# Four units of a gated convolution multiply behind the gathered rows, in quarters instead of halves

## The reference

```
h = np.maximum(x @ w_in, 0.0)                 # x: (2, 768, 384), w_in: (384, 1024)
conv_out[t] = sum over k of conv_w[k] * h[t + k - 1]     # 3 taps, zero-padded
gate = 1.0 / (1.0 + np.exp(-conv_out))
out  = (h * gate) @ w_out                     # w_out: (1024, 384)
```

## Time and profile before

| | us |
|---|---|
| median of 3 runs | 523.26 (516.58 to 534.95) |
| the profiled execution | 522.37 |
| its span, first to last instruction | 520.9 |
| TensorE busy in the span | 484.9 (93%) |
| DVE, ACT, POOL busy | 375.4, 288.2, 82.4 |

### The profile page before, as it was taken

How to read it: one execution, slowest core, us unless ns; L and a number is a source line. 1 busy time by engine, 2 the same in 40 slices (tenths; PEclk the granted TensorE clock), 3 DMA queues, 4 the chain that set the end, 5 groups by cost and what they waited for, 6 DMA issues and landing times.

```text
span 520.9 us, 15282 instructions
## 1 busy us (share of the span) xinstructions
PE 484.9 (93%) x6083; PEld 424.1 (81%) x6083; DVE 375.4 (72%) x606; ACT 288.2 (55%) x469; POOL 82.4 (16%) x121
## 2 busy tenths in 40 slices
PE   8979999999999888899999999999986699999997
PEld 4548888687677657799989989999876689999997
DVE  6887787676024344999999999999875467789661
ACT  4513443241123241999899899898853254444543
POOL 6622232020201121010010110100004400000000
PEclk9979999799579688899999999999997799999999
DMA  7672301022420105485476476430163300000202
GB/s 142 119 135 41 65 6 35 4 53 82 143 81 19 49 30 183 152 287 190 149 271 209 151 254 213 164 107 30 62 226 89 109 0 1 2 0 1 91 2 91
DMA packets 59275, 52.58 MB, mean 101 GB/s; under 512 B 41395, under 2 KB 52275, under 8 KB 59094
## 3 DMA queue, kind: packets, MB, share of 16 engines
q1 hardware_dynamic: 53142, 39.21, 26.0%
q0 software_dynamic: 3968, 12.19, 6.8%
q10 hardware_dynamic: 2112, 0.39, 0.4%
HBM read 77.74 MB, written 10.22 MB: 169 GB/s over the span
## 4 chain that ended last, share of the span: by engine, by line
PE 81%; DVE 6%; SPq 4%; issue 4%; DMA 2%; ACT 2%; another core or an unknown queue 1%; DVEq 0%; ACTq 0%
PE ps L1916 5%; PE ps L1918 5%; PE ps L1917 5%; PE ps L1130 5%; PE ps L1934 5%; PE ps L1933 5%; PE ps L1935 5%; PE ps L2199 3%; PE ps L2201 3%; PE ps L2213 3%; PE ps L2214 3%; PE ps L2215 3%; PE ps L2200 3%; PE ps L1291 3%; PE ps L1925 3%
## 5 line engine op out<-in xcount | busy, mean ns | idle before, releaser
L1837 DVE TENSOR_TENSOR w2l<-raw,w2h 128x768 fp32r<-128x768 f32 x76 | 67.7, 953 | 6.8 <-ACT w2h L1770 6.8
L1837 DVE TENSOR_TENSOR w1l<-raw,w1h 128x1024 fp32r<-128x1024 f32 x57 | 66.4, 1220 | 6.3 <-ACT w1h L1770 4.3
L1770 ACT CAST w1h<-raw 128x1024 fp32r<-128x1024 f32 x57 | 56.4, 1063 | 4.7 <-DMA raw<-in_moe_w_dram 4.7
L1770 ACT CAST w2h<-raw 128x768 fp32r<-128x768 f32 x76 | 58.1, 848 | 0.2 <-DMA raw<-in_moe_w_dram 0.2
L1933 PE MATMUL ps<-w2h,hh 128*128 128x384 f32 x152 | 52.4, 345 | 1.6 <-DVE hl L1842 1.6
L1935 PE MATMUL ps<-w2h,hl 128*128 128x384 f32 x152 | 50.9, 335 | 0.0
L1934 PE MATMUL ps<-w2l,hh 128*128 128x384 f32 x152 | 50.8, 334 | 0.0
L1130 PE MATMUL ps<-idle_b 128*128 128x512 bf16 (+3 forms) x160 | 47.1, 402 | 1.9 <-DVE idle_b L765 1.8
L1916 PE MATMUL ps<-w1h,xh 128*128 128x512 f32 x114 | 47.0, 412 | 0.6 <-DVE xl L1829 0.6
L1918 PE MATMUL ps<-w1h,xl 128*128 128x512 f32 x114 | 45.2, 397 | 0.0
L1917 PE MATMUL ps<-w1l,xh 128*128 128x512 f32 x114 | 44.8, 393 | 0.0
(11 more groups left out here) (232 smaller groups left out, 1046.5 us busy)
## 6 DMA issues: line engine op xcount, KB each, us to landing
raw<-in_moe_w_dram SPq DMA_DIRECT2D x54, 512.0 KB
raw<-in_moe_w_dram SPq DMA_DIRECT2D x72, 384.0 KB
x_all<-x_sorted POOLq DMA_DIRECT2D x19, 192.0 KB, 2.9
y_sorted<-x_all POOLq DMA_DIRECT2D x19, 192.0 KB, 2.6
raw<-in_q_dram SPq DMA_DIRECT2D x24, 96.0 KB, 3.0
v_nat<-in_v_dram SPq DMA_DIRECT2D x24, 96.0 KB, 3.0
out_dram<-res SPq DMA_DIRECT2D x12, 192.0 KB, 1.9
raw<-in_k_dram SPq DMA_DIRECT2D x20, 96.0 KB, 3.0
```

Of the source, the lines that this page charges most:

```text
L1770: act.copy(hi(par), raw).then_inc(s_wh, 1)
L1837: dve.tensor_tensor(lo(par), raw, hi(par).bitcast(F32), ALU.subtract).then_inc(s_wl, 1)
```

## The change

The first four units make their first products in quarters of the positions (3 blocks, 192 columns) instead of halves (6 blocks, 384 columns). The quarter of blocks 0 to 2 is multiplied behind the transposes of blocks 3 (units 0 and 1), 4 (unit 2) and 5 (unit 3); the quarter of blocks 3 to 5 behind 6, 6, 7 and 8; that of blocks 6 to 8 behind 9, 9, 10 and 11; the last one after the last block. ACT's order follows. Units 4 to 15 keep their halves.

```
-    NS = NSTEP // NCH
...
-        CHUNKS = [(i, j) for j in range(NCH) for i in range(LAG)] + [(i, j) for i in range(LAG, NU) for j in range(NCH)]
+
+        PARTS = [slice(n, n + NSTEP // 4) for n in range(0, NSTEP, NSTEP // 4)]
+        HALVES = [slice(n, n + NSTEP // 2) for n in range(0, NSTEP, NSTEP // 2)]
+        CHUNKS = [(i, r) for r in PARTS for i in range(LAG)] + [(i, r) for i in range(LAG, NU) for r in HALVES]
...
-        FIRST = {NS - 1: (0,), NS: (1,), NS + 2: (2,), NSTEP - 1: (3,)}
-
-        def chunk(i, j):
-            return CHUNKS.index((i, j))
+        BEHIND = {n: [] for n in range(NSTEP)}
+        for p in range(3):
+            for i, n in enumerate((0, 0, 1, 2)):
+                BEHIND[PARTS[p].stop + n].append((i, PARTS[p]))
+
+        def chunk(i, r):
+            return CHUNKS.index((i, r))
+
+        def last_chunk(i):
+            return max(k for k, c in enumerate(CHUNKS) if c[0] == i)
...
-                act.activation(h[:, i % NH, 1 + j * CW:1 + (j + 1) * CW], psH[chunk(i, j) % NCH],
-                               ACT.Relu).then_inc(s_hs, 1)
+                act.activation(h[:, i % NH, 1 + r.start * STEP:1 + r.stop * STEP],
+                               psH[chunk(i, r) % NCH][:, 0:(r.stop - r.start) * STEP], ACT.Relu).then_inc(s_hs, 1)
...
             for n in range(NSTEP):
                 high_x(n)
-                for i in FIRST.get(n, ()):
-                    relu(i, 0)
-            relu(0, 1)
-            relu(1, 1)
+                for i, r in BEHIND[n]:
+                    relu(i, r)
+            relu(0, PARTS[-1])
+            relu(1, PARTS[-1])
             for i in range(NU):
                 sigmoid(i)
                 if i == 0:
-                    relu(2, 1)
-                    relu(3, 1)
+                    relu(2, PARTS[-1])
+                    relu(3, PARTS[-1])
...
             for n in range(NSTEP):
                 turn(n)
-                if n == NS - 1:
+                if n == PARTS[0].stop:
                     pe.wait_ge(s_cc, 1)
-                    pe.wait_ge(s_ml, NS)
-                for i in FIRST.get(n, ()):
-                    up(i, 0)
+                for i, r in BEHIND[n]:
+                    pe.wait_ge(s_ml, r.stop)
+                    up(i, r)
             pe.wait_ge(s_ml, NSTEP)
             for i in range(LAG):
-                up(i, 1)
+                up(i, PARTS[-1])
             for i in range(LAG, NU + LAG):
                 if i < NU:
-                    for j in range(NCH):
-                        up(i, j)
+                    for r in HALVES:
+                        up(i, r)
                 down(i - LAG)
```

More of the change, by code:

```diff
@@ L2060, in high_x, with relu @@
                 act.copy(mh[:, n].rearrange("p c b t -> p (c b t)"), psM[n % NM]).then_inc(s_mh, 1)
-            def relu(i, j):
-                act.wait_ge(s_hp, chunk(i, j) + 1)
-                if i >= NH and j == 0:
+            def relu(i, r):
+                act.wait_ge(s_hp, chunk(i, r) + 1)
+                if i >= NH and r.start == 0:
                     act.wait_ge(s_gg, i - NH + 1)
-                act.activation(h[:, i % NH, 1 + j * CW:1 + (j + 1) * CW], psH[chunk(i, j) % NCH],
-                               ACT.Relu).then_inc(s_hs, 1)
+                act.activation(h[:, i % NH, 1 + r.start * STEP:1 + r.stop * STEP],
+                               psH[chunk(i, r) % NCH][:, 0:(r.stop - r.start) * STEP], ACT.Relu).then_inc(s_hs, 1)
             def sigmoid(i):
@@ L2098, in _ @@
                 if i == 0:
-                    relu(2, 1)
-                    relu(3, 1)
+                    relu(2, PARTS[-1])
+                    relu(3, PARTS[-1])
                 if i in (12, 13, 14):
-                    for j in range(NCH):
-                        relu(AFTER_GATE[i], j)
+                    for r in HALVES:
+                        relu(AFTER_GATE[i], r)
                 high(i)
                 if i in AFTER_GATE and i < 12:
-                    for j in range(NCH):
-                        relu(AFTER_GATE[i], j)
+                    for r in HALVES:
+                        relu(AFTER_GATE[i], r)
                 if i == STORES_AFTER:
@@ L2127, in conv_first @@
                     dve.wait_ge(s_sg, i - 1)
-                dve.wait_ge(s_hs, chunk(i, NCH - 1) + 1)
+                dve.wait_ge(s_hs, last_chunk(i) + 1)
                 dve.tensor_scalar(cv[:, i % 2], h[:, i % NH, 0:S], cw[:, units[i][1], 0:1], None,
@@ L2187, in turn, with up @@
                 t.then_inc(s_mt, 1)
-            def up(i, j):
+            def up(i, ns):
                 b, f = units[i]
                 fs = slice(f * P, (f + 1) * P)
-                ns = slice(j * NS, (j + 1) * NS)
-                k = chunk(i, j)
-                o = psH[k % NCH].rearrange("p (n t) -> p n t", t=STEP)
+                k = chunk(i, ns)
+                o = psH[k % NCH][:, 0:(ns.stop - ns.start) * STEP].rearrange("p (n t) -> p n t", t=STEP)
                 if k >= NCH:
```

## The result

The change made the kernel slower: 530.27 us (median of 4 runs, 526.66 to 535.70) against 522.96 (4 runs, 516.58 to 534.95), a ratio of **1.0216 [1.0153, 1.0279]**. Both limits lie above 1, so it is slower; whether by more than 2% they do not decide. The forecast was 521.3, about nothing. A repetition with four more runs gave 1.0125 [1.0035, 1.0215]. The ratios leave out the runs with a disturbed clock, which the medians here contain, and so they are not the quotients of these medians. So a stretch of the third layer, which repeated to 0.2 us in two traces of each kernel, is the better instrument and is used throughout.

A forecast was written before the change was run, and what follows sets the result against it. TensorE, under way for 93% of the span, was taken as the bound, so unit 4's start decided. Quarters, transposes and waits moved it 1.1 us earlier: span 520.9 - 1.1 = 519.8, plus 1.5, 521.3 us; range 516 to 554.

The forecast's parts named there:

- A quarter's matmul, 0.115: TensorE's 192-column products: spacing bound by the weight load, 0.115 us each, 1.035 a quarter against 1.59 a half.
- wide-cost: Rival for TensorE's quarters: each narrow product costs as much as a wide one, 0.1766 us; time 527, chance 0.10.
- column-bound: Rival for TensorE's quarters: columns bind and loads hide, 0.096 us a matmul; time 519, chance 0.07.
- f32-rate: Rival for TensorE's quarters: narrow products run at the plain f32 rate, 0.36 us each; time 553, chance 0.22.
- The first quarter 8.24 after the first gather: Start of the block stretch: first quarter at about 404.45 in place of 409.43, behind block 3's transposes.
- The last quarters 24.6 after the first gather: End of the block stretch: 404.45 + 12.4 quarters + 2.4 transposes + 1.5 waits puts the last quarters at 420.8.
- a ReLU with its latency is 0.6: Two-bank rule on TensorE: the ReLU's 0.6 us hides under a whole quarter, 1.035, so costs nothing.
- 1.5 us of waits for remainders: TensorE in the block stretch: added waits for remainders of blocks 5, 8 and 11, 0.4 + 0.4 + 0.7 us.
- a paragraph for the low clock: Block stretch, outside the sum: 6.7 us at half speed lose up to 3.3; unit 4 at 427.8 to 429.8.
- The end of the stretch, 5.6 us from the last quarters to unit 4, 1.5 of it idle: Last quarters to unit 4's start at 426.4: TensorE idles 1.5 us until relu(2), behind the sigmoid.
- The tail unchanged at 90.2: From unit 4's first product to the last matmul: TensorE stays full, the 90.2 us are moved and not shortened.
- The sum: Whole kernel: unit 4 starts 1.1 us earlier, 427.50 to 426.4; span 519.8 plus 1.5 around it, 521.3.

The follow-up runs named there:

- e2: Changed kernel with POOL's twelve indirect gathers replaced by plain row loads from SP's queue; stretch 34.55 us, time 525.96 us, no ratio.
- e5: Changed kernel with the indirect gathers replaced by plain row loads issued by POOL; stretch 37.46 us, ratio to the kernel before 1.0009 [0.9955, 1.0064].
- e9: The kernel before run once more, no edit, for a second trace; stretch 37.90 us, one run, 514.82 us.
- e4: Kernel before plus 18 unused 192-column matmuls behind block 3's transposes, among the gathers; stretch 43.92 us, ratio to before 1.0039 [0.9955, 1.0124].
- e1: The changed kernel once more, no edit; stretch 44.25 us, ratio to the kernel before 1.0125 [1.0035, 1.0215].

## Why the prediction was wrong

*A quarter's matmul, 0.115*: right. They are 0.111 apart at full clock (nine from 403.85 to 404.85) and 0.213 at the lower one (0.21 from 410.11 to 410.32), so the wide-cost, the column-bound and the f32-rate rivals all fall, the last with its 0.22. By the page "TensorE: Matmul & The Clock Gate" of the Trainium skill, section "Back-to-back issue gap", N / 2.4 plus 2.5 ns would be 82 ns for an isolated matmul; the page adds that this under-counts at small N, where the weight load is left out, and the trace's 111 agrees with that.

*The first quarter 8.24 after the first gather* (404.45 less 396.21): right, 402.90 less 394.57 is 8.33.

*The last quarters 24.6 after the first gather*: this is **the step that failed**: the stretch of the blocks, summed with prompt signals and at full clock. They start at 426.13, 31.56 after it, 7.0 late. Two of its terms took signals to be prompt: "a ReLU with its latency is 0.6" against the quarter that it hides under, put among the costs taken at nothing, and 1.5 us of waits for remainders, with copies 0.6 to 1 us behind their transposes. The runs showed ReLUs 4.2 and 6.8 us behind the last matmul's start, and a copy 7.0 behind its transposes. The 7.0 divide so:

- idle time 4.0 in place of 1.5: +2.5;
- the lower clock. TensorE is busy for 8.33 us at 0.50, work that takes about 4.3 at the upper level (0.111 for 0.213): +4.0;
- the first matmul behind a block's transposes or a wait takes 0.17 and not 0.11, in some ten products: +0.6;
- 108 matmuls 0.004 closer than forecast: -0.4.

That is 6.7 of 7.0, by estimates from the rows. Whether the second term follows from the first is not shown. Here the clock falls at 407.4, when TensorE has done nothing since 405.4, and comes back at 417.6; in e2, with every signal in time, it stays at 1.00 from 412 to unit 4. But e5's clock falls with every signal in time, and of the two traces of the kernel before the first has a low stretch of 6.8 us with TensorE busy for 3.80, and e9's has this one:

```profile
395.60:405.90 10.30, 7.69 (x27) 6.36 (x26) 4.65 (x9) 2.41 (x5) 6.20 (x7) 0.50 0.54 153
```

It is as long and nearly as busy as after's 10.20 and 8.33, in a layer stretch of 37.90. So a low clock that costs some 3.4 us (an estimate: 7.69 us of work, with wide matmuls 0.32 apart for 0.1766) belongs to the kernel before as well, and the term says what the full-speed sum left out rather than what parts the two kernels. The prediction had a paragraph for the low clock, outside its sum, with "up to 3.3" lost; that term was near, and late signals come on top of it.

*The end of the stretch, 5.6 us from the last quarters to unit 4, 1.5 of it idle*: right. 426.13 to 431.77 is 5.64; these rows of ACT in the kernel after show relu(0), the sigmoid and relu(2) with relu(3), answering to the earlier trace rows:

```profile
427.42 0.33 ACT L2074 ACTIVATE h<-ps 128x192 f32<-128x192 f32 x1 [1.10 <-PE ps L2208]
...
430.65 0.85 ACT L2081 ACTIVATE raw<-cv 128x768 f32<-128x768 f32 x1 [0.59 <-DVE cv L2143]
431.40 0.53 ACT L2074 ACTIVATE h<-ps 128x192 f32<-128x192 f32 x2
```

A ReLU of 192 columns is 0.33 as taken, and TensorE's wait of 1.37 ends with relu(2). *The tail unchanged at 90.2*: right, 90.15.

*The sum*: unit 4 was to start 30.2 after the first gather and starts 37.20 after it; before it was 31.29. So +5.9 stands for -1.1, and "what is late is TensorE itself" was true in a way that the sum missed: late in reporting. The chance on the slower side, 0.22, sat on a mechanism that did not occur; that the result came out there is no credit to it.

**The clue was in the trace.** The prediction read block 4's path, 2.2 us, as slow "during the gathers" and went on. Before's trace had the next block worse. Here are its transposes on TensorE and its copy on ACT, in the kernel before:

```profile
406.23 0.90 PE L2186 MATMUL ps<-ident,x_all 128*128 128x128 f32 x3 [0.70 <-DVE x_all L2118]
```

```profile
408.26 0.48 ACT L2060 CAST mh<-ps 128x384 fp32r<-128x384 f32 x1 [1.67 <-PE ps L2186]
```

The copy is 2.03 behind, where block 11's was 0.59 behind in the quiet stretch (419.65). Some of the 2.03 is the transposes themselves, at the lower clock, but more than a microsecond of the 2.30 that TensorE idles in the earlier trace rows was this. In e9 the same copy was in time and TensorE idled for 1.21 there, so in the kernel before, too, the held signal differs from one execution to the next. In the attention stage, where POOL also runs indirect transfers, before's chain of waits holds a piece that names no engine:

```profile
166.69 3.27 another core or an unknown queue
```

The kernel runs on one core, so there is no other to wait for. The kernel after has the same at the same place: ACT's copy at 170.05 stands behind 4.09 us of idle put down to "remote". Both figures are ACT's idle time; the product that it copies (L1250) was over about 1.6 us before the copy in the kernel before and 2.4 in the kernel after.

**What stays open.** By what path the signals are held was not tried, nor whether any other traffic as long as the gathers, from SP or POOL, would hold them too. Nor was it tried whether they are held when nothing is recorded. That rival is untested: TensorE's instructions and the semaphore updates are themselves recorded, and of the updates some are missing from the traces during the gathers (in e9, 7 stand for the 12 blocks' transposes; with plain loads all 12 are there). Every run counted here has a span and a granted clock from such records, so the agreement of the whole times with the stretches (+5.9 us is 1.1%, the repeat's ratio 1.0125) does not settle it. What of the first ratio, 2.2%, lies beyond the layer's 1.1% is not explained. Why exactly some signals pass (408.10, during the gathers) and others wait for their end is open too.

## What to carry to other kernels

Idle time of TensorE beside indirect transfers is not free room: before filling it, compare there, signal by signal, the start of each consumer with the start of the last instruction it waits for, and take the distance from that stretch and not from a quiet one. A wait that the profile puts down to "remote" or "issue", on one core, ahead of an instruction whose inputs are long ready, is such a late signal. Such a bracket holds the engine's whole idle time, of which only a part is lateness. And a schedule with two banks turns one late signal into idle TensorE, here 3.08 us until the first ReLU. The lower clock is a price of its own, which a sum at full speed leaves out.

## What the runs showed of the hardware

- What TensorE had finished was seen by ACT up to 7.1 us behind the instruction's start while POOL's indirect gathers ran (e4; 0.6 is usual) and 0.5 to 0.6 us after the last traffic in three executions: 411.1 and 411.68 (after), 417.9 and 418.36 (e1), 420.2 and 420.67 (e4). It is TensorE's semaphore update that is recorded late, and held updates come in a burst and in order (420.59, 420.64, 420.70 in e4). With the same blocks loaded plainly, from SP's or POOL's queue, no such delay was seen, but those loads were over at 416.6 (e2), before two quarters had run, and at 404.1 (e5), when one had.
- The length depended on how densely TensorE had issued: 9, 18 narrow matmuls and 12 wide ones lengthened the stretch by 3.6, 5.8 and 2.5 us, and the 18 ahead of the gathers by 0.1.
- A matmul of 192 columns of this type, each with its own weights, takes 0.111 us at the upper clock and 0.213 at the lower, against 0.1766 for 384 columns at the upper one: halving the columns saves 37%, not half.
